# Quarter-array products of the queries with the attention state, and a new order at both edges of the experts' stage

## The reference

```python
# 1 decay attention: q, k, v are 2 x 8 heads x 768 x 64, in blocks of 64 positions
intra = einsum('bhij,bhjd->bhid', (qb @ kb.T) * lam ** (i - j), vb)      # i >= j
inter = einsum('bhid,bhde->bhie', qb * lam ** (i + 1), kv_state)
out = intra + inter
kv_state = lam ** block * kv_state + (kb * lam ** (block - 1 - i)).T @ vb
# 2 mixture of experts on x = 1536 tokens x 512: 8 experts, top 1
e = argmax(x @ w_gate); gate = softmax(x @ w_gate)[e]
x = gate * (maximum(x @ w1[e], 0) @ w2[e])       # w1 512 x 1024, w2 1024 x 512
# 3 dense layer: w_in 512 x 2048, w_out 2048 x 512
h = x @ w_in
return (h - tanh(h)) @ w_out
```

## Time and profile before

| | us |
|---|---|
| median of 3 runs (lowest, highest) | 537.2 (536.25, 538.38) |
| the profiled execution, its own time | 537.62 |
| the profiled execution, span from first to last instruction | 535.8 |
| attention, about | 0 to 63 |
| routing and gathers, about | 63 to 78 |
| experts | 78 to 262 |
| dense layer | 263 to the end |

### The profile page before, as it was taken

How to read it: one execution, slowest core, us unless ns; L and a number is a source line. 1 busy time by engine, 2 the same in 40 slices (tenths; PEclk the granted TensorE clock), 3 DMA queues, 4 the chain that set the end, 5 groups by cost and what they waited for, 6 DMA issues and landing times.

```text
span 535.8 us, 11128 instructions
## 1 busy us (share of the span) xinstructions
PE 512.1 (96%) x3994; PEld 456.1 (85%) x3995; DVE 361.6 (67%) x542; ACT 262.6 (49%) x485; POOL 318.2 (59%) x261
## 2 busy tenths in 40 slices
PE   5999979989999999999899999999999999999994
PEld 4999879989999999999788888888888888888883
DVE  7555455644546455445199999979987765998781
ACT  1344516556656656666364545454434343443431
POOL 4866057535455455454388989876855553875542
PEclk9999999989999999999999999999999999999998
DMA  8897648467687787775350000001100000100002
GB/s 319 274 302 235 196 119 269 145 222 227 202 235 207 224 235 195 235 231 164 126 209 1 2 0 1 1 0 40 39 2 1 1 0 0 60 20 2 0 1 78
DMA packets 32411, 64.57 MB, mean 121 GB/s; under 512 B 3696, under 2 KB 7792, under 8 KB 32368
## 3 DMA queue, kind: packets, MB, share of 16 engines
q1 hardware_dynamic: 30448, 57.71, 34.8%
q0 software_dynamic: 1920, 6.29, 3.6%
HBM read 57.69 MB, written 6.29 MB: 119 GB/s over the span
## 4 chain that ended last, share of the span: by engine, by line
PE 90%; DVE 3%; ACT 2%; DMA 2%; issue 1%; POOL 1%; SPq 0%; ACTq 0%; POOLq 0%; DVEq 0%
PE bank L321 27%; PE bank L323 26%; PE bank L322 26%; PE bank L1170 2%; PE bank L1145 2%; PE bank L1156 2%; PE bank L1191 1%; PE bank L1253 1%; PE bank L1182 1%; PE bank L1198 1%; DMA wst<-in_w_dram 1%; DMA x_sorted<-token_rows,tokid 1%; PE bank L1343 1%; POOL w_l L622 0%; POOL out_dram L663 0%
## 5 line engine op out<-in xcount | busy, mean ns | idle before, releaser
L622 POOL TENSOR_TENSOR w_l<-wst,w_h 128x512 fp32r<-128x512 f32 x64 | 87.1, 1361 | 85.0 <-ACT w_h L743 84.5
L671 POOL TENSOR_SCALAR big<-h_sq 128x512 uint8<-128x512 f32 x48 | 80.4, 1674 | 36.9 <-ACT h_sq L824 36.6
L685 POOL TENSOR_TENSOR g_l<-g,g_h 128x512 fp32r<-128x512 f32 x46 | 61.2, 1329 | 42.8 <-ACT g_h L834 42.8
L321 PE MATMUL bank<-xs_h,w_h 128*128 (+1 forms) x256 | 71.1, 278 | 5.0 <-DVE w_l L1025 3.4
L321 PE MATMUL bank<-wo_h,g_h 128*128 128x512 f32 x192 | 75.5, 393 | 0.1
L323 PE MATMUL bank<-wo_l,g_h 128*128 128x512 f32 x192 | 75.1, 391 | 0.0
L322 PE MATMUL bank<-wo_h,g_l 128*128 128x512 f32 x192 | 74.6, 389 | 0.0
L323 PE MATMUL bank<-x_l,win_h 128*128 128x512 f32 x188 | 74.3, 395 | 0.0
L321 PE MATMUL bank<-x_h,win_h 128*128 128x512 f32 x188 | 73.9, 393 | 0.0
L322 PE MATMUL bank<-x_h,win_l 128*128 128x512 f32 x188 | 73.7, 392 | 0.0
L321 PE MATMUL bank<-h_h,w_h 128*128 128x232 f32 x256 | 71.1, 278 | 0.7 <-POOL w_l L622 0.7
(11 more groups left out here) (151 smaller groups left out, 1106.7 us busy)
## 6 DMA issues: line engine op xcount, KB each, us to landing
wst<-in_w_dram SPq DMA_DIRECT2D x128, 256.0 KB
qk_in<-in_qk_t_dram SPq DMA_DIRECT2D x12, 512.0 KB, 6.0
kv_in<-in_kv_dram SPq DMA_DIRECT2D x12, 512.0 KB, 4.9
win<-in_w_in_dram SPq DMA_DIRECT2D x8, 512.0 KB, 5.0
wo<-in_w_out_dram SPq DMA_DIRECT2D x8, 512.0 KB, 7.8
token_rows<-x_sb SPq DMA_DIRECT2D x12, 256.0 KB, 4.5
x_sorted<-token_rows,tokid POOLq DMA_INDIRECT x12, 4.4
out_dram<-rows,tokid POOLq DMA_INDIRECT x12
```

The lines of the kernel that those rows point to most:

```text
L321: pe.matmul(dst, lh, rh, start=start, stop=False, skip_group_check=True)
L622: pool.tensor_tensor(w2_l[:, j % STG], wst2[:, j % STG], w2_h[:, j % 2].bitcast(F32), ALU.subtract).then_inc(w2l_ready, 1)
L671: pool.tensor_scalar(big[:, f % 2], h_sq[:, f % 2], T * T, None, ALU.is_ge).then_inc(big_ready, 1)
L685: pool.tensor_tensor(g_l[:, f % 2], g[:, f % 2], g_h[:, f % 2].bitcast(F32), ALU.subtract).then_inc(gl_ready, 1)
```

## The change

Five edits. (1) `old_outputs` splits every product over the column halves too, so that it works on quarters of the array: 16 matmuls with 64 stationary columns for 8 with 128. (2) In expert 0 the split of `w_in` moves from step 7 to step 4, on ACT and on DVE. (3) In expert 0 `turn(LATER[j])` stands ahead of `first_product(j + 2)`. (4) In expert 7 `first_product(7)` stands behind `second_product(5)`, so that it lies between the last two second products. (5) The last output of the experts leaves PSUM in two halves, the first as soon as the last `second_product` has finished its first two of four k, and `hidden2_first` takes its matmuls by k.

```diff
@@ ACT, expert
-                    if j == (JT - 1 if first else 3):
+                    if j == (4 if first else 3):
                         act.wait_ge(wi_in, 16 * e + 16)
                         act.copy(win_h[...], win[...]).then_inc(winh_ready, 1)
@@ ACT, after the experts
-            y_out(JT * E, act.value_load(...), (E - 1) % 2, E - 1)
+            off = act.value_load(off_i[0:1, E - 1:E], min_val=0, max_val=N)
+            ge(act, y_low_ready, E - 1)
+            act.wait_ge(last_half_done, 1)
+            act.copy(x2_h[:, k_halves[0], bass.ds(off, WIN)], psYs[(E - 1) % 2][:, k_halves[0]]).then_inc(last_half_high, 1)
+            act.wait_ge(second_done, JT * E)
+            act.copy(x2_h[:, k_halves[1], bass.ds(off, WIN)], psYs[(E - 1) % 2][:, k_halves[1]]).then_inc(y_high_ready, 1)
@@ DVE: the same two edits, with last_half_high, last_half_low, y_high_ready and y_low_ready
...
@@ PE, old_outputs
                     for a, rows64 in halves:
-                        pe.matmul(psO[:, a, p * D:(p + 1) * D], q_dec[rows64, t % 2, p, :], state[rows64, t % B, p, :],
-                                  start=p == 0, stop=False, skip_group_check=True)
+                        for half, cols64 in halves:
+                            pe.matmul(psO[cols64, a, p * D:(p + 1) * D], q_dec[rows64, t % 2, p, cols64],
+                                      state[rows64, t % B, p, :], start=p == 0, stop=False, skip_group_check=True)
@@ PE, second_product
+                    if tell_half and k == KT // 2 - 1:
+                        i.then_inc(last_half_done, 1)
@@ PE, expert
                 for j in range(JT):
+                    if first:
+                        turn(LATER[j])
                     if j + 2 < JT:
-                        first_product(off, j + 2, JT * e + j + 2)
+                        if not (last and j + 3 == JT):
+                            first_product(off, j + 2, JT * e + j + 2)
...
-                    if first:
-                        turn(LATER[j])
-                    second_product(j, JT * e + j, side)
+                    second_product(j, JT * e + j, side, tell_half=last and j == JT - 1)
+                    if last and j + 3 == JT:
+                        first_product(off, j + 2, JT * e + j + 2)
@@ PE, hidden2_first
-            pe.wait_ge(y_high_ready, E)
-                for part in range(3):
-                    if part == 2:
-                        pe.wait_ge(y_low_ready, E)
-                    for k in range(KT):
-                        i = pe.matmul(bank[:, 0, :], (win_h, win_l, win_h)[part][:, k, 0:P],
-                                      (x2_h, x2_h, x2_l)[part][:, k, 0:CHUNK], ...)
+                pe.wait_ge(last_half_high, 1)
+                for k in range(KT):
+                    if k == KT // 2:
+                        pe.wait_ge(y_high_ready, E)
+                    for w in (win_h, win_l):
+                        pe.matmul(bank[:, 0, :], w[:, k, 0:P], x2_h[:, k, 0:CHUNK], ...)
+                pe.wait_ge(last_half_low, 1)
+                pe.wait_ge(y_low_ready, E)
+                for k in range(KT):
+                    i = pe.matmul(bank[:, 0, :], win_h[:, k, 0:P], x2_l[:, k, 0:CHUNK], ...)
```

More of the change, by code:

```diff
@@ L271, in decay_attention_moe_kernel @@
         hl_ready = sem("hl_ready")
+        last_half_done = sem("last_half_done")
+        last_half_high = sem("last_half_high")
+        last_half_low = sem("last_half_low")
         y_high_ready = sem("y_high_ready")
@@ L797, in _ @@
             n_ov = experts(act, expert)
-            y_out(JT * E, act.value_load(off_i[0:1, E - 1:E], min_val=0, max_val=N), (E - 1) % 2, E - 1)
+            off = act.value_load(off_i[0:1, E - 1:E], min_val=0, max_val=N)
[4 more added lines that the diff above has]
+            act.copy(x2_h[:, k_halves[1], bass.ds(off, WIN)], psYs[(E - 1) % 2][:, k_halves[1]]).then_inc(y_high_ready, 1)
             with act.If(n_ov > 0):
@@ L1074, in _ @@
             n_ov = experts(dve, expert)
-            y_out(E, dve.value_load(off_i[0:1, E - 1:E], min_val=0, max_val=N), (E - 1) % 2)
+            off = dve.value_load(off_i[0:1, E - 1:E], min_val=0, max_val=N)
+            dve.wait_ge(last_half_high, 1)
+            dve.tensor_tensor(x2_l[:, k_halves[0], bass.ds(off, WIN)], psYs[(E - 1) % 2][:, k_halves[0]],
+                              x2_h[:, k_halves[0], bass.ds(off, WIN)].bitcast(F32), ALU.subtract).then_inc(last_half_low, 1)
+            dve.wait_ge(y_high_ready, E)
+            dve.tensor_tensor(x2_l[:, k_halves[1], bass.ds(off, WIN)], psYs[(E - 1) % 2][:, k_halves[1]],
+                              x2_h[:, k_halves[1], bass.ds(off, WIN)].bitcast(F32), ALU.subtract).then_inc(y_low_ready, 1)
             with dve.If(n_ov > 0):
@@ L1273, in first_product, with second_product @@
                 i.then_inc(first_done, 1)
-            def second_product(j, unit, side, begun=False):
+            def second_product(j, unit, side, begun=False, tell_half=False):
                 pe.wait_ge(w2l_ready, unit + 1)
@@ L1334, in _ @@
             pe.wait_ge(winl_ready, E)
-            pe.wait_ge(y_high_ready, E)
             def hidden2_first():
-                for part in range(3):
-                    if part == 2:
-                        pe.wait_ge(y_low_ready, E)
-                    for k in range(KT):
-                        i = pe.matmul(bank[:, 0, :], (win_h, win_l, win_h)[part][:, k, 0:P],
-                                      (x2_h, x2_h, x2_l)[part][:, k, 0:CHUNK], start=part == 0 and k == 0,
-                                      stop=part == 2 and k == KT - 1, skip_group_check=True)
+                pe.wait_ge(last_half_high, 1)
[3 more added lines that the diff above has]
+                    for w in (win_h, win_l):
+                        pe.matmul(bank[:, 0, :], w[:, k, 0:P], x2_h[:, k, 0:CHUNK], start=w is win_h and k == 0, stop=False,
+                                  skip_group_check=True)
+                pe.wait_ge(last_half_low, 1)
+                pe.wait_ge(y_low_ready, E)
+                for k in range(KT):
+                    i = pe.matmul(bank[:, 0, :], win_h[:, k, 0:P], x2_l[:, k, 0:CHUNK], start=False, stop=k == KT - 1,
+                                  skip_group_check=True)
                 i.then_inc(hidden_done, 1)
```

## The result

| | before | after |
|---|---|---|
| median of 20 runs (lowest, highest), us | 537.87 (535.41, 541.55) | 533.08 (529.91, 539.0) |
| ratio of the two, 95% interval | | 0.9912 (0.9889 to 0.9934) |
| the profiled execution, its own time | 537.62 | 531.83 |
| its span | 535.8 | 530.0 |

The change makes the kernel 0.9% faster, more than the 0.5% that a measurement can tell. 533.4 was predicted. Where the 5.8 lie is read from five places on PE in both traces: its start, the first record of the group of state and q, the last of the logits, the first product, the first matmul of the dense stage.

The account below looks back on a forecast made before the run. PE was taken to bound the kernel, with time to win only at the edges of the experts' stage. -4.46 - 0.5 - 0.71 - 1.05 + 2.9 = -3.8 gave 533.4 us against the median 537.2; range 528.4 to 535.2.

Parts of the forecast that it names:

- Release: Edit 2, expert 0: SP no longer held by the late w_in copy, next w1 part arrives before PE asks; -4.46 us.
- Turns: Edit 3, expert 0: idle before units 2 and 8 filled, but waits for gathered rows come; -0.5 us, between -2.0 and +0.4.
- The last expert: Edit 4: a product now lies in between, so PE's wait for POOL's last w_l goes; -0.71 us.
- the halved output: Edit 5, edge to the dense stage: the first half is copied sooner, PE begins at 262.42, not 263.47; -1.05 us.
- Quarters: Edit 1, attention loop: group of state and q takes 1.23 us instead of 0.94; +2.9 us over ten tiles.
- Sixteen of the one are then 0.93: Attention q group: sixteen 64-column matmuls take 0.93 us, eight 128-column ones 0.90, so the split itself gains nothing.
- The 0.15 at the group's end: Attention q group: cost of the change of tiling at its end, 0.15 us, part of the forecast 1.23.
- the 0.10 at the scores' end: Attention, scores before the q group: added cost of a change of tiling, 0.10 us, part of the forecast 1.23.
- The rival of four at once: Attention q group: four quarters load together, group 0.80 to 0.81 us, ten of them -1.3, time 529.2; chance 0.28.
- single quarters: Attention q group: quarters load one after another, +1.22 us a tile, +12.2, time 542.7; chance 0.05.
- late gathers with a slow clock: Expert 0: both landings at 5.2, slow matmuls cost 1.7 us again, turns' term +0.4, time 536.0; chance 0.07.
- the held SP: Expert 0: something else in SP's fixed order holds it, the 4.46 us stay, time 537.8; chance 0.04.

Follow-up runs that it names:

- the clean loop: Changed kernel with only an eighth of q, k and v loaded from tile 4 on; attention 41.83 us, as against 44.27 without edit 1.
- quarters alone: Edit 1 alone on the kernel before; ratio 1.0034 (1.0012 to 1.0056), attention 46.50 us.
- late weights and without quarters: Change without edit 1, SP's loads of the first expert's weights and w_in moved behind the last store of x; ratio 0.99 (0.987 to 0.993).
- light loads: Changed kernel, with and without edit 1, loading only an eighth of q, k and v from tile 4 on; attention 41.83 us with, 44.27 without.
- release alone: Edit 2 alone on the kernel before; ratio 0.9936 (0.9913 to 0.9958).
- quarters by column: Changed kernel with the loop over column halves outermost in the q products; ratio 0.9921 (0.9899 to 0.9944), group 0.91 us.

## Why the prediction came out as it did

The time was right, 533.1 for 533.4, and so were the direction and most of the steps. One step, the cost of the group on quarters, was wrong in its sign, and a cost that was not foreseen hid that.

- **Release, -4.46: right.** The eight products took 10.72, SP did not pause, the clock stayed. Alone it brings 3.8, since unit 8 then begins 0.5 later.
- **Turns, -0.5: mis-sized.** Unit 8 began 24.00 after the first product, 25.30 before: -1.30. The waits forecast for tiles 8 and 10, 0.8 and 0.65, were 0 and about 0.15; in their place tile 6, for which the term has no wait, cost an idle time of 0.43, 0.65 from start to start. The term held POOL's gathers at their old times. POOL also waits for ACT's w_h, which came sooner: counted from the first product, the gather of tile 8 went out at 9.32 where it had been 9.85, and that of tile 10 at 13.03 where it had been 13.55. PE, held up at tile 6, asked for both 0.65 later.
- **The last expert, -0.71, and the halved output, -1.05: right.** The gap of 0.71 is gone; 0.20 is left of 1.20, so -1.00. The halves took 0.55 each, as estimated from 0.93 and 0.36 by columns.
- **Quarters, +2.9: wrong.** Two sizes in it failed. "Sixteen of the one are then 0.93" comes near only for the other order of the loops (0.91); with four different quarters in a row the group is 0.62, its ends included. The 0.15 at the group's end did not come on top: outputs, gate and update kept their 0.98, 0.44 and 0.59. Only the 0.10 at the scores' end came, as the Trainium skill's drain at a change of mode (TensorEngine Tiling (Array Packing), Key Properties) has it. Even two at a time would have cost 0.91 + 1.09 against 0.94 + 0.99, +0.07 a tile, not 0.29.
- **The rival of four at once, 0.28, was the true one** for the group. It was held down by the argument that no group gets below 0.027 us for a record. But each of those groups works on at most two parts of the array, so they had no say on four. It says eight rounds of four records, and eight rounds they are; but by the order of the program the four records of a round are two matmuls, on two quarters and not on four. Its grounds were off as well: it took the halves to "work two at a time" from the 0.112 of the earlier trace rows, but those matmuls are fp32r with 232 moving columns and say nothing of an fp32 record of 128. In the kernel before no two matmuls of the program start together on halves. 32 records in 0.62 are 0.019 each. The Trainium skill's floor of 25 ns from start to start (TensorE: Matmul & The Clock Gate, section "Wait — 56ns, not 53.3ns?") does not hold for this group, neither on the mean nor inside a round of four, 7 ns apart, if a record is an instruction, as the count of 256 has it. The two records of each fp32 matmul start 7 ns apart in the kernel before too. The rival's price was -1.3, the clean loop gives -2.4.
- **Not foreseen: late instructions.** The sum priced an added instruction by PE's time for it, and not by its 64 bytes that have to arrive. The kernel before had a first sign, 0.30 of idle at 48.77 with no releaser and 0.84 in its whole attention stretch (45.11 against 44.27), and the block has become shorter than the packet's way under full load. It also brought the slow clock once, in quarters alone. Net of what was there before: -2.4 + 4.4 - 0.8 = +1.1 for +2.9.
- **The first 19 us, +0.68**, lie ahead of any group the change touches. The two runs with the change and without quarters have 18.70 and 18.57 there, the one with late weights and without quarters 19.99, so it goes with the execution.

Sum for the traces: -7.6 + 1.1 + 0.7 = -5.8, against -3.8; the medians give -4.8. That the time was met to 0.3 us is luck in two places. The group on quarters was priced 5.3 too dear (+2.9 for -2.4), and 3.6 of late instructions that nobody had priced cancel most of it. And the 1.0 by which the change of the medians exceeds the forecast is mostly made up by the start: 537.2 was the median of three runs, and over twenty the kernel before has 537.87. The rivals of single quarters, of late gathers with a slow clock and of the held SP are refuted by the rows above.

Open is what delays the packet: that it starts late when the DMA engines are full is shown, whether it waits in its own queue or behind the data on the engines was not tried. Nor was a change of 2 and 3 together.

## What to carry to other kernels

Small matmuls on quarters of the array can overlap, but it hangs on which quarter follows which: the same sixteen took 0.62 in one order of the loops and 0.91 in the other. Price the group by a run of its own order, not by a rate of halves. A faster group is not yet a faster kernel, though: every instruction is also 64 bytes of a stream in blocks of 256: where a loop becomes denser and the DMA engines are full, count how long a block lasts and look for idle times of PE without a releaser, in the middle of a group. And cost a moved order with the moved queue behind it: when PE's steps come sooner, so do the helpers that wait for them.

## What the runs showed of the hardware

- PE's instructions come in packets of 16 KB. With a DMA share of 0.84 (15 to 43 us of the changed kernel) the next one started 1.6 to 3.3 us after PE had passed a boundary, over all runs up to 4.6; under light loads (share 0.24) 0.3 to 1.0. PE goes on 1.0 to 1.6 after the packet's end. Stops without a releaser, 0.03 to 1.93 us, came in the attention loops only at places that are multiples of 256 instructions apart.
- A plain fp32 matmul of the program has two records. One with 128 stationary columns takes 0.112 (scores, state and q before), one with 64 takes 0.058 (outputs, gate, update, quarters by column), with four different quarters in a row 0.029. Halves of the rows or of the columns alone showed no gain beyond the smaller load: outputs alternate the column halves on all rows, and still take 0.058 each. On quarters two column neighbours start together, by the order of the program, and the next two 0.058 later; three rounds of the other order also hold two, and which pairs can is open.
- The clock is no sure function of idle times: 0.72 and 1.20 within 3 us were followed by a mean of 0.83 in one execution (release alone), and by 1.00 in the kernel before; a stop of 1.93 was followed by 0.57 over 4 us (quarters alone), one of 1.81 by 1.00 (quarters by column).
